# ScalarE scales six of twelve tiles, and VectorE's step takes the last low parts first and the next row maximum last

## What is computed

```python
q_bits = (np.einsum('bhsd,dk->bhsk', q, proj) > 0)      # the same for k; bucket = bits as a number
mask = q_bucket[:, :, :, None] == k_bucket[:, :, None, :]
scores = np.where(mask, scale * np.matmul(q, k.transpose(0, 1, 3, 2)), -1000000000.0)
scores = scores - np.max(scores, axis=-1, keepdims=True)
attn = np.exp(scores)
attn = attn / (np.sum(attn, axis=-1, keepdims=True) + 1e-09)
x = np.matmul(attn, v)                                   # 2 x 8 heads, 768 x 768, head size 64
x = ((x @ w1) * (x @ w2)) @ w3 @ w_out                   # 1536 tokens, 512 -> 1024 -> 1024 -> 512
out = (1 / (1 + np.exp(-(x @ w_gate))) * (x @ w_val)) @ w2_out   # 512 -> 1536 -> 512
```

## Time and profile before

| | us |
|---|---|
| median of 3 runs (774.24 to 775.75) | 775.24 |
| the profiled execution, its time | 775.34 |
| its span | 773.3 |
| TensorE busy | 731.5 (95%) |
| VectorE busy | 480.9 (62%) |
| ScalarE busy | 456.2 (59%) |
| GpSimd busy | 345.2 (45%) |

### The profile page before, as it was taken

How to read it: one execution, slowest core, us unless ns; L and a number is a source line. 1 busy time by engine, 2 the same in 40 slices (tenths; PEclk the granted TensorE clock), 3 DMA queues, 4 the chain that set the end, 5 groups by cost and what they waited for, 6 DMA issues and landing times.

```text
span 773.3 us, 12684 instructions
## 1 busy us (share of the span) xinstructions
PE 731.5 (95%) x4136; PEld 675.3 (87%) x4136; DVE 480.9 (62%) x1032; ACT 456.2 (59%) x842; POOL 345.2 (45%) x253
## 2 busy tenths in 40 slices
PE   6798989899898989799999999999999999999998
PEld 4687878778797878799999999999999999988886
DVE  5899999999999999832432833624324326774100
ACT  5788888897888988545446424564454454715100
POOL 3867364554628697164466600054653554140000
PEclk9999999999999999999999999999999999999999
DMA  5774443436273500001001000010010010401001
GB/s 154 219 175 105 116 124 94 129 89 165 71 175 91 115 12 18 28 28 56 28 27 54 1 0 1 1 55 28 28 54 28 27 55 0 163 1 68 28 28 41
DMA packets 26609, 51.79 MB, mean 67 GB/s; under 512 B 4161, under 2 KB 12689, under 8 KB 26577
## 3 DMA queue, kind: packets, MB, share of 16 engines
q1 hardware_dynamic: 26272, 51.32, 24.4%
q10 hardware_dynamic: 304, 0.07, 0.0%
HBM read 29.43 MB, written 3.15 MB: 42 GB/s over the span
## 4 chain that ended last, share of the span: by engine, by line
PE 74%; DVE 13%; issue 6%; ACT 4%; DMA 2%; SPq 1%; DVEq 0%; ACTq 0%
PE pair_bank L1296 14%; PE pair_bank L1298 14%; PE pair_bank L1297 13%; PE bank L1296 5%; PE bank L1298 5%; PE bank L1297 5%; PE bank L1224 5%; PE bank L1209 5%; PE pair_bank L1197 4%; DVE pt_lo L957 4%; DVE rowmax L924 4%; ACT pt_hi L617 2%; DMA qk_raw<-in_qk 2%; DVE prob L949 1%; PE bank L1258 1%
## 5 line engine op out<-in xcount | busy, mean ns | idle before, releaser
L1062 DVE TENSOR_TENSOR u<-bank,u 128x384 f32<-128x384 f32 x80 | 44.3, 555 | 135.5 <-ACT u L617 126.6
L617 ACT ACTIVATE u<-pair_bank 128x384 f32<-128x384 f32 x120 | 58.7, 491 | 109.3 <-PE pair_bank L1298 109.1
L1209 PEld LDWEIGHTS bank<-ident,prob 128*128 128x128 f32 x576 | 65.8, 141 | 49.7 <-DVE pt_lo L957 29.7
L1209 PE MATMUL bank<-ident,prob 128*128 128x128 f32 x576 | 85.3, 281 | 24.9 <-DVE pt_lo L957 24.3
L617 ACT ACTIVATE pt_hi<-bank 128x384 fp32r<-128x384 f32 x192 | 85.8, 489 | 32.2 <-PE bank L1209 31.7
L957 DVE TENSOR_TENSOR pt_lo<-bank,pt_hi 128x384 fp32r<-128x384 f32 x192 | 97.4, 548 | 7.8 <-ACT pt_hi L617 7.5
L650 ACT ACTIVATE prob<-pair_bank,ebias,escale 128x768 f32<-128x768 f32 x96 | 95.1, 991 | 7.2 <-DVE ebias L935 7.0
L924 DVE TENSOR_REDUCE rowmax<-pair_bank 128x1 f32<-128x768 f32 x96 | 90.9, 947 | 4.2 <-PE pair_bank L1197 4.0
L1197 PE MATMUL pair_bank<-mk,sq 128*128 128x384 f32 x384 | 89.7, 356 | 3.6 <-ACT prob L650 1.9
L1296 PE MATMUL pair_bank<-y_hi,g_hi 128*128 128x384 f32 x240 | 80.3, 335 | 0.0
L1197 PEld LDWEIGHTS pair_bank<-mk,sq 128*128 128x128 f32 x384 | 65.2, 191 | 8.8 <-issue 6.2
(11 more groups left out here) (162 smaller groups left out, 1953.6 us busy)
## 6 DMA issues: line engine op xcount, KB each, us to landing
sq<-hl SPq DMA_DIRECT2D x45, 192.0 KB
mk<-hl SPq DMA_DIRECT2D x15, 384.0 KB
qk_raw<-in_qk SPq DMA_DIRECT2D x7, 768.0 KB, 5.6
w_raw<-in_w SPq DMA_DIRECT2D x16, 256.0 KB, 2.7
v_raw<-in_v SPq DMA_DIRECT2D x16, 192.0 KB, 2.7
wo_raw<-in_wo SPq DMA_DIRECT2D x12, 256.0 KB, 3.6
out<-out_sb SPq DMA_DIRECT2D x12, 256.0 KB, 2.0
mk<-hl SPq DMA_DIRECT2D x15, 192.0 KB
```

The costliest lines, as they stand in the source:

```text
L617: return act.activation(dst, src, ACT.Copy)
L1209: mm = pe.transpose(t_bank[j][:, 128 * t:128 * t + 128], prob[k % 3][:, 128 * (3 * j + t):128 * (3 * j + t) + 128], ident[:, :])
```

## The change

- NORM_ON_ACT is (2, 3, 5, 8, 9, 11) and compared with the step itself: steps 3 and 9 are scaled by ScalarE as well.
- VectorE's step is in another order.
- At the seam: both parts of B22 are made by GpSimd, behind the last scores; T4's sum is begun before the attention ends, in a half by VectorE (`x_sum4_begin`), with a copy by ScalarE of the half of T2 that is needed later (`x_take_t2`); VectorE makes the low parts of T2, T1 and B21 in another order, and ScalarE their high parts.

```diff
@@ -53,7 +53,7 @@
 SCALE = 1.0 / float(np.sqrt(D))
 PEN = float(2 ** 30)
 WARM = (10, 30)
-NORM_ON_ACT = (2,)
+NORM_ON_ACT = (2, 3, 5, 8, 9, 11)
 
 
 
@@ -67,9 +67,8 @@
 BLK = 256
 SUM_AT = {T1: 1, T3: 2, T2: 3, T4: 4}
 LOW_ORDER = (B11, T3, T1, B22, T2, B21, T4)
-X_HI_ORDER = ((T2, 0), (T2, 1), (T1, 0), (T1, 1), (B22, 0), (B21, 0), (B22, 1), (T4, 0), (B21, 1), (T4, 1))
-X_LOW_ORDER = ((T3, 0), (T3, 1), (T2, 0), (T1, 0), (T2, 1), (T1, 1), (B22, 0), (B22, 1), (B21, 0), (B21, 1),
-               (T4, 0), (T4, 1))
+X_HI_ORDER = ((T2, 0), (T2, 1), (T1, 0), (T1, 1), (B21, 0), (B21, 1), (T4, 0), (T4, 1))
+X_LOW_ORDER = ((T3, 0), (T3, 1), (T2, 0), (T2, 1), (T1, 0), (T1, 1), (B21, 0), (B21, 1), (T4, 0), (T4, 1))
 PAIRS1, PAIRS3 = KF // 2, KF2 // 2
 
 
@@ -244,6 +243,7 @@
         w_ready = [sem("w_ready0"), sem("w_ready1")]
         fill_half, rows_set = sem("fill_half"), [sem("rows_set0"), sem("rows_set1")]
         x_sums_done, x_sum4_done = sem("x_sums_done"), sem("x_sum4_done")
+        x_sum4_begun, x_t2_taken = sem("x_sum4_begun"), sem("x_t2_taken")
         x_hi_early, x_low_early = sem("x_hi_early"), sem("x_low_early")
         x_hi_done, x_ready = sem("x_hi_done"), sem("x_ready")
         h_hi_done, h_ready = sem("h_hi_done"), sem("h_ready")
@@ -566,6 +566,14 @@
                     pool.wait_ge(s_done, STEPS * (PAIRS - 1) + QT)
                     for side in range(2):
                         rounded(x_high(T3, side), x_raw(T3, side)).then_inc(x_hi_early, 1)
+                    pool.wait_ge(s_done, STEPS * PAIRS)
+                    for side in range(2):
+                        rounded(x_high(B22, side), x_raw(B22, side)).then_inc(x_hi_early, 1)
+                    for side in range(2):
+                        pool.wait_ge(x_hi_early, side + 5)
+                        pool.wait_ge(x_sums_done, side + 5)
+                        pool.tensor_tensor(x_low(B22, side), x_raw(B22, side), x_high(B22, side).bitcast(F32),
+                                           ALU.subtract).then_inc(x_low_early, 1)
                 if ahead:
                     pair_sums_low(0, 0)
 
@@ -630,7 +638,7 @@
 
             def x_operand_high(q, side):
 
-                if q in (T1, B22):
+                if q == T1:
                     act.wait_ge(s_done, STEPS * PAIRS)
                 if q in (T2, T1):
                     act.wait_ge(x_sums_done, {T2: 3, T1: 5}[q] + side)
@@ -639,8 +647,15 @@
                     act.wait_ge(wp_done, PAIRS)
                     act.wait_ge(x_done, 2 * PAIRS - 1 + 2 * side)
                 if q == T4:
+                    act.wait_ge(x_sum4_begun, 1)
                     act.wait_ge(x_sum4_done, side + 1)
                 copy(x_high(q, side), x_raw(q, side)).then_inc(x_hi_done, 1)
+
+            def x_take_t2():
+
+                act.wait_ge(x_sums_done, 4)
+                act.wait_ge(wp_done, PAIRS)
+                copy(x_sums[T4][0][:, :, 1, :], x_sums[T2][0][:, :, 1, :]).then_inc(x_t2_taken, 1)
 
             def exp(p, k):
 
@@ -688,7 +703,7 @@
                         transposed_hi(p, k - 1)
                     elif not first:
                         transposed_hi(p - 1, STEPS - 1)
-                    if k % UQ in NORM_ON_ACT:
+                    if k in NORM_ON_ACT:
                         act.wait_ge(rnorm_done, s + 1)
                         act.activation(prob[k % 3][:, :], prob[k % 3][:, :], ACT.Copy,
                                        scale=rnorm[:, k:k + 1]).then_inc(norm_done[k % UQ], 1)
@@ -788,23 +803,22 @@
                 for go, *args in behind_last:
                     go(*args)
 
+            x_take_t2()
             kept1(0, 0, 0, u_x)
             pair_raw_high(1, 1)
             kept1(0, 0, 1, u_x)
+            x_operand_high(T1, 1)
             attention_halves(3, PAIRS - 1, keep=False)
-            x_operand_high(T1, 1)
-            x_operand_high(B22, 0)
+            kept2(0, 0, 0, u_x)
             x_operand_high(B21, 0)
-            kept2(0, 0, 0, u_x)
-            x_operand_high(B22, 1)
             kept2(0, 0, 1, u_x)
+            x_operand_high(B21, 1)
             kept4(0, 0, 0, u_x)
+            kept4(0, 0, 1, u_x)
             x_operand_high(T4, 0)
-            kept4(0, 0, 1, u_x)
-            x_operand_high(B21, 1)
-            gate(ACT.Copy, 0, 0, y4_mm, 0, 0, y_bank[0], g12_done)
             x_operand_high(T4, 1)
-            gate(ACT.Copy, 0, 1, y4_mm, 0, 0, y_bank[1], g12_done)
+            for side in range(2):
+                gate(ACT.Copy, 0, side, y4_mm, 0, 0, y_bank[side], g12_done)
             pair_sums_high(1, 1)
             gates_but_first(ACT.Copy, 0, u_x)
             act.wait_ge(wp_done, PAIRS)
@@ -949,9 +963,9 @@
                 dve.tensor_scalar(prob[k % 3][:, :], prob[k % 3][:, :], rnorm[:, k:k + 1], None,
                                   ALU.mult).then_inc(norm_done[k % UQ], 1)
 
-            def transposed_lo(p, k):
+            def transposed_lo(p, k, halves=(0, 1)):
                 s = STEPS * p + k
-                for j in range(2):
+                for j in halves:
                     dve.wait_ge(pt_hi_done, 2 * s + j + 1)
                     cut = (slice(None), slice(3 * j, 3 * j + 3), slice(128 * (k % UQ), 128 * (k % UQ) + 128))
                     dve.tensor_tensor(pt_lo[(k // UQ) % 2][cut], t_bank[j][:, 0:384].rearrange("p (t n) -> p t n", t=3),
@@ -969,19 +983,30 @@
                     dve.wait_ge(x_sums_done, 3 + side)
                 else:
                     dve.wait_ge(x_hi_done, X_HI_ORDER.index((q, side)) + 1)
-                if q in (T2, B21):
+                if q == T2:
+                    dve.wait_ge(x_sums_done, 5 + side)
+                    dve.wait_ge(x_sum4_begun, 1)
+                    dve.wait_ge(x_t2_taken, 1)
+                if q == B21:
+                    dve.wait_ge(x_sum4_begun, 1)
                     dve.wait_ge(x_sum4_done, side + 1)
-                if q in (T2, B22):
-                    dve.wait_ge(x_sums_done, 5 + side)
                 dve.tensor_tensor(x_low(q, side), x_raw(q, side), x_high(q, side).bitcast(F32),
                                   ALU.subtract).then_inc(x_ready, 1)
 
+            def x_sum4_begin():
+
+                dve.wait_ge(x_done, 2 * (PAIRS - 1))
+                dve.wait_ge(x_sums_done, 4)
+                dve.wait_ge(wp_done, PAIRS)
+                dve.tensor_tensor(x_sums[T4][0][:, :, 0, :], x_f[:, PAIRS - 2, :].rearrange("p (s n) -> p s n", s=2),
+                                  x_sums[T2][0][:, :, 0, :], ALU.subtract).then_inc(x_sum4_begun, 1)
+
             def x_sum4(side):
 
+                late = x_sums[T4][0][:, side, 1, :]
                 dve.wait_ge(x_done, 2 * PAIRS - 1 + 2 * side)
-                dve.wait_ge(x_sums_done, 3 + side)
-                dve.wait_ge(wp_done, PAIRS)
-                dve.tensor_tensor(x_raw(T4, side), x_raw(B21, side), x_raw(T2, side),
+                dve.wait_ge(x_t2_taken, 1)
+                dve.tensor_tensor(late, x_f[:, PAIRS - 1, HALF * side:HALF * side + HALF], late,
                                   ALU.subtract).then_inc(x_sum4_done, 1)
 
             def code(p):
@@ -998,20 +1023,19 @@
             def pair(p, first=False, last=False):
                 for k in range(STEPS):
                     nxt = None if last and k == STEPS - 1 else (p, k + 1) if k + 1 < STEPS else (p + 1, 0)
+                    last_step = (p, k - 1) if k > 0 else (p - 1, STEPS - 1)
+                    sum_eps(p, k)
+                    if k > 0 or not first:
+                        transposed_lo(*last_step, (0,))
+                    inverse(p, k)
+                    if k > 0 or not first:
+                        transposed_lo(*last_step, (1,))
+                    if k not in NORM_ON_ACT:
+                        normalise(p, k)
                     if nxt:
                         row_max(*nxt)
-                    sum_eps(p, k)
-                    if nxt:
                         exp_scale(*nxt)
-                    inverse(p, k)
-                    if nxt:
                         exp_bias(*nxt)
-                    if k % UQ not in NORM_ON_ACT:
-                        normalise(p, k)
-                    if k > 0:
-                        transposed_lo(p, k - 1)
-                    elif not first:
-                        transposed_lo(p - 1, STEPS - 1)
                     if k == 2 and not last:
                         code(p + 1)
                     if last and k == STEPS - 1:
@@ -1042,18 +1066,20 @@
                 pair(p)
             pair(PAIRS - 1, last=True)
             transposed_lo(PAIRS - 1, STEPS - 1)
-            dve.wait_ge(x_done, 2 * (PAIRS - 1))
+            x_sum4_begin()
+            x_operand_low(T2, 0)
+            x_operand_low(T2, 1)
             dve.wait_ge(x_kept, 4 * PAIRS - 1)
             attention_out(slice(0, 2 * D), 0, x_f[:, PAIRS - 1, 0:HALF])
             x_sum4(0)
-            x_operand_low(T2, 0)
             x_operand_low(T1, 0)
+            x_operand_low(T1, 1)
```

(6 more changed lines are left out.)

## The result

| | before | after |
|---|---|---|
| median, us | 775.5 (4 runs) | 934.86 (4 runs, 934.56 to 935.57) |
| ratio | | 1.2043 (95%: 1.2017 to 1.2069) |
| span of the profiled execution | 773.3 | 933.2 |

The account below looks back on a forecast made before the run. The prediction took VectorE's work to bound the kernel before, and a serial loop through VectorE and ScalarE after. 775.3 us, plus 179 to the last exponential, less 4 at the seam, gave 950, range 922 to 998.

Parts of the forecast that it names:

- The loop: Attention steps: VectorE's new order and each exponential wait for each other in turn; 58.1 us a pair against 35.5.
- The plain step: One attention step with nothing added, from one exponential's start to the next: 4.07 us, twelve to a pair.
- The two copies: Copies of attention output between exponential and high parts in steps 1, 4, 7 and 10: 0.98 us each time.
- VectorE's scalings: Scalings left on VectorE in steps 0, 1, 4, 6, 7 and 10: 0.80 us each, ends 0.62 and 0.93.
- the product bank: Its copy, once a pair in the attention, adds 0.50 us.
- The sum: Delay to the last exponential: +21.5 us in pair 0, +134.4 in six pairs, +23.5 in pair 7, together +179.
- ScalarE's scalings and TensorE: Attention steps: ScalarE's six scalings, 0.94 us each, are hidden; TensorE's scores, values and fill also fit.
- The seam: From attention to the first layer unit: most of 5.5 us of TensorE loss removed; -4 us, ends -6 and +7.
- The clock: Rival: TensorE's clock falls to 1.2 GHz in the attention; 1010 us if low throughout, 980 if half; chance 0.15.
- The faster rival: VectorE is limited by work, its order makes no difference, and moving two scalings gains: 756 us; chance 0.02.
- the shorter loop: Rival: attention copies covered, 31 us less in all, and VectorE's scalings undisturbed: about 905 us; chance 0.06.
- The rule by operation count: Skill's advice to minimize operation count: VectorE's two fewer operations per pair would gain up to 15 us; prediction went against it.

Follow-up runs that it names:

- two runs: Kernel before with steps 3 and 9 also scaled by ScalarE: 781.31 us; kernel with the new seam alone, ScalarE scaling 3, 4, 8 and 11: 775.43 us.

## Why the prediction was right

- **The loop.** Read from the order and priced from the first tile, where the same operations happened to run one behind the other. The pair was forecast at 58.1 us and took 56.1. The plain step was given 4.07 and took 3.91: the exponential to the high part is 0.98, and only where the two copies come first it is 1.11; my one row pair was of the second kind. That is 0.12 us too much in two steps of three, and the other 0.04 is in the low parts and the maximum. The two copies with their later start cost 1.15 instead of 0.98.
- **VectorE's scalings** have a mean of 0.79 us (40 of them in 80 to 450 us), as interpolated, but on the path each costs 0.67 (the rest of the 56.14 us between exponentials: 46.92 for twelve plain steps, 4.6 for copies, 0.48 for the product bank, 0.1 at the loop's end, divided by six), since the maximum begins before the scaling has ended, 0.52 after its start where it is undisturbed. This term was sized from a place where 0.63 passed.
- **The sum**: +179 to the last exponential, measured +164.8; of the 14 us, 15 lie in the plain steps (0.16 times 95), 6 in the scalings, and the copies take 5 back; the 2 us that this is too much went to what was not priced. Pair 0 ended at 71.86, forecast 73.9.
- **ScalarE's scalings and TensorE** are hidden, as forecast: transposes waited for VectorE's scaling, but exponentials for nothing but the bias.
- **The seam**: -4 forecast, -4.9 measured, of which the run with the seam alone shows 2 to 3. No wait above 1 us was left.
- **Rivals.** The clock did fall, which I had given 0.15. In step 1 TensorE waits for 2.74 us and not for under 2: I had put its bits of the next pair into that wait, and they run before it.

```profile
250.14 1.54 PE L1235 MATMUL bank<-ident,prob 128*128 128x128 f32 x6 [2.74 <-DVE prob L963]
...
250.00:252.00 2.00, 1.86 (x8) 1.87 (x9) 1.24 (x4) 0.65 (x1) 2.00 (x2) 0.50 0.00 0
```

  The last line is the busy time of 250 to 252 us, at a granted clock of 0.50, the lower level of 1.2 GHz. From 254 us on it was at 1.00 again, and the fall cost nothing: a pair at 0.94 and a pair at 1.00 both take 56.13 us. The price that I gave to this rival was for a clock that stays down, and the pairs after pair 0 have a mean of 0.94 or more. The page "TensorE: Matmul & The Clock Gate" of the Trainium skill, section "HAM oscillation — how this bites in real kernels", has the clock fall at every one of a kernel's repeated waits and charges the kernel for it. The trace agrees in part: the pair from 296.41 has the same wait of 2.74 us and stays at 1.00, and where the clock fell nothing was lost. The faster rival is excluded by the runs with the added maximum; the shorter loop by the 1.15 us of the copies. The rule by operation count would have had the maximum behind the bias cost as much as the one ahead of it: 0 against 84 us.
- **Wrong, and outside the sum**: the prediction said that VectorE's work bounds the pair before, from the exponential's short waits for its bias. It did not ask what TensorE waits for. TensorE's work and its waits for low parts make up the pair, and VectorE's busy time fell by over 0.9 us in two runs, with the pair 0.15 us shorter in one and 0.2 longer in the other. For the same reason the two scalings, taken for a gain if all else stayed, gain nothing in the old order: that kernel is about 5 us slower, in pairs at a lower clock. None of this entered the sum, since the loop replaces that bound, but it was the price of the faster rival, whose 756 us are not reached by any run here.

## What to carry to other kernels

When a step's order is changed on one engine, follow one value around all engines and back, and add up starts, not durations: what counts is whether something long stands between giving out a value and asking for what comes of it. The same instruction was free at one place and cost 84 us at another, and busy times per pair said nothing of it. The wait of an instruction for another engine's operation does not go by taking that instruction away: look at what starts next under the same operation, and at whether the engine that sets the pace waits behind it. A scaling of 1.3 us in step 3 brought TensorE a wait of 1.02 us, and one as long in step 10 a wait of 0.2.

## What was new about the hardware

- VectorE's scaling of 128x768 in place (0.62 us alone) ends 0.41 to 0.43 us after a GpSimd operation under which it started, whatever it had already waited: 1.34, 1.60 and 2.60 us in the rows above, and so do 24 scalings of the trace of before. Two that started in the last 0.1 us of such an operation took 0.62 us. The row maximum, which reads PSUM, took 0.944 to 0.958 us in all 96 cases of the changed kernel, GpSimd busy or not.
- The clock falls too in a kernel whose pace TensorE sets, and there it costs. Of two pairs with equal work, one took 35.38 us at 1.00 and one 36.94 at 0.95. The run with the old order shows the same in one of these three pairs. TensorE waited 1.77 us for low parts ahead of that fall, but it waited 1.74 at the same place of the pair in the first row, which has none: the wait alone does not decide it.

```profile
88.94:124.31 35.37, 32.88 (x201) 28.59 (x201) 33.58 (x92) 31.69 (x64) 17.66 (x13) 1.00 0.47 119
124.31:161.28 36.97, 34.42 (x202) 30.13 (x201) 33.66 (x92) 31.67 (x65) 17.67 (x13) 0.95 0.45 114
161.28:196.67 35.39, 32.87 (x202) 28.56 (x201) 33.59 (x92) 31.66 (x65) 17.66 (x13) 1.00 0.47 119
```
